# Causal attention with a convolved and a mixing feed-forward block: one-piece eviction of even heads, earlier inversion, held-back last products, one tap on ScalarE

## What is computed

```
cum    = cumsum(max(s, 0))
scores = q k^T / 8 + min(-(cum_i - cum_j), 0), causal mask, minus the row's maximum
x      = exp(scores) / (sum(exp(scores)) + 1e-9) @ v      heads side by side: 576 x 512
h      = relu(x @ w_in)                                    512 -> 1024
c      = conv_w[0]*h[t-1] + conv_w[1]*h[t] + conv_w[2]*h[t+1]
x1     = (h * sigmoid(c)) @ w_out                          1024 -> 512
u      = x1 + (U V)^T x1 over positions                    rank 32
out    = u + relu(u @ w_ch1) @ w_ch2                       512 -> 2048 -> 512
```

## Time and profile before

| | |
|---|---|
| median of 3 runs | 909.75 us (909.56 to 910.51) |
| profiled execution, its own time | 910.62 us |
| its span | 908.8 us |
| PE busy | 861.6 us, 95% |
| DVE, ACT, POOL busy | 468.5, 372.5, 50.6 us |
| granted clock of PE, mean | 0.992 |
| DMA | 150.36 MB, 165 GB/s |

### The profile page before, as it was taken

The page is one execution under the profiler, slowest core; times in us unless marked ns, Lnnn a source line. Parts: engine busy times, 40 slices in busy tenths (PEclk is TensorE's granted clock), DMA queues, the critical chain, the costliest instruction groups (busy, mean ns, idle before and its releaser), DMA issues.

```text
span 908.8 us, 15655 instructions
## 1 busy us (share of the span) xinstructions
PE 861.6 (95%) x6184; PEld 809.2 (89%) x6184; DVE 468.5 (52%) x984; ACT 372.5 (41%) x709; POOL 50.6 (6%) x105
## 2 busy tenths in 40 slices
PE   4888898989999999999999999999999999999998
PEld 3666888879998999889998999988999999999998
DVE  6788694464445934555344871455323761442222
ACT  2777675554425634544332653444221431221110
POOL 3021000000000000000000000000000000000000
PEclk9999998989999999999999999999999999999999
DMA  7686945636663557336545454435444444274441
GB/s 162 164 228 157 305 141 189 222 73 199 214 209 104 188 167 259 127 106 212 180 152 177 129 172 145 134 100 184 146 145 169 141 174 150 94 240 182 150 175 53
DMA packets 64396, 150.36 MB, mean 165 GB/s; under 512 B 30026, under 2 KB 44362, under 8 KB 51780
## 3 DMA queue, kind: packets, MB, share of 16 engines
q1 hardware_dynamic: 61252, 144.50, 49.4%
q0 software_dynamic: 3072, 4.87, 2.1%
HBM read 119.15 MB, written 30.11 MB: 164 GB/s over the span
## 4 chain that ended last, share of the span: by engine, by line
PE 66%; DVE 13%; issue 10%; ACT 5%; DMA 4%; POOL 1%; SPq 1%; DVEq 0%; ACTq 0%; POOLq 0%
PE psum L1190 18%; PE psum L1192 18%; PE psum L1191 17%; PE psum L1169 5%; DVE work L958 2%; DVE psum L899 2%; PE psum L1116 2%; DVE work L961 2%; DMA few_scratch<-few 2%; PE psum L1148 2%; PE psum L1146 2%; DMA spread_out<-few_scratch 2%; DVE work L956 1%; ACT work L746 1%; DVE ybuf L973 1%
## 5 line engine op out<-in xcount | busy, mean ns | idle before, releaser
L1190 PE MATMUL psum<-r_hl,ring 128*128 128x288 f32 x512 | 153.6, 300 | 3.2 <-DVE r_hl L1001 1.7
L1190 PE MATMUL psum<-uu_hl,ring 128*128 128x288 f32 x512 | 153.2, 299 | 1.5 <-DVE r_hl L1001 1.5
L1192 PE MATMUL psum<-r_hl,ring 128*128 128x288 f32 x512 | 151.2, 295 | 0.0
L1191 PE MATMUL psum<-r_hl,ring 128*128 128x288 f32 x512 | 151.1, 295 | 0.0
L1192 PE MATMUL psum<-uu_hl,ring 128*128 128x288 f32 x512 | 151.0, 295 | 0.0
L1191 PE MATMUL psum<-uu_hl,ring 128*128 128x288 f32 x512 | 150.9, 295 | 0.0
L783 ACT ACTIVATE r_hl<-psum 128x288 fp32r<-128x288 f32 x128 | 52.5, 411 | 188.1 <-PE psum L1192 188.0
L1001 DVE SCALAR_TENSOR_TENSOR r_hl<-psum,r_hl 128x288 fp32r<-128x288 f32 x128 | 58.5, 458 | 134.7 <-ACT r_hl L783 134.6
L1169 PE MATMUL psum<-probs,va 128*65 128x320 f32 (+4 forms) x448 | 109.6, 364 | 6.5 <-ACT probs L694 6.3
L899 DVE CUSTOM_DVE_ANT_0 psum<-psum,key_late 128x512 f32<-128x512 f32 (+4 forms) x160 | 84.9, 564 | 57.1 <-PE psum L1116 56.8
L1190 PEld LDWEIGHTS psum<-r_hl,ring 128*128 128x128 f32 x512 | 96.6, 189 | 5.5 <-DVE u_acc L1013 2.7
(11 more groups left out here) (101 smaller groups left out, 1626.6 us busy)
## 6 DMA issues: line engine op xcount, KB each, us to landing
ring<-w_scratch SPq DMA_DIRECT2D x74, 1024.0 KB, 4.9
w_scratch<-ring SPq DMA_DIRECT2D x24, 1024.0 KB, 6.1
kq_raw<-in_kq_t SPq DMA_DIRECT2D x64, 288.0 KB, 5.0
stage<-in_w_ch SPq DMA_DIRECT2D x16, 512.0 KB, 4.7
spread_out<-few_scratch POOLq DMA_DIRECT2D x32, 144.0 KB, 3.2
out_t<-u_acc SPq DMA_DIRECT2D x16, 288.0 KB, 3.7
va<-in_v SPq DMA_DIRECT2D x32, 128.0 KB, 2.8
stage<-in_w_out SPq DMA_DIRECT2D x4, 512.0 KB, 6.5
```

The lines of the kernel that those rows point to most:

```text
L1190: pe.matmul(o, hi, m_hi, start=start, stop=False)
L1191: pe.matmul(o, hi, m_lo, start=False, stop=False)
L1192: return pe.matmul(o, lo, m_hi, start=False, stop=stop)
```

## The change

Four parts.

1. **Eviction.** The even head's 65 rows are evicted in one instruction, with a bias column `eps_col` that holds 1e-9 in row 64 alone. Its sums then lie in row 64 of `x_raw`, which belongs to the odd head's half, and are gathered from there. So the odd head's ACT copy into `x_raw` now waits until the even head's gather has landed (`few_in`, 16 of 32). The odd head's gather waits for that too. At the steps of `EVICT_LATE` the eviction stands behind the group's feed-forward items.
2. **Inversion.** The last pair of batches 1 to 3 is inverted at the end of its own head 7, and for batches 1 and 2 normalised and split one step sooner. In batches 1 to 3 pair 1 is normalised at head 6, g = 1 instead of head 5, g = 3, and split at head 7 instead of head 6.
3. **Last products.** The first wi, wo and up of a batch do all tiles but the last for both halves, then the last tile of half 0, then (as the second item) that of half 1.
4. **Middle tap.** In batch 0 ACT makes the middle tap, right behind the second half of `hidden`; DVE makes the outer two.

```diff
-        X_SPLIT = [{(5, 0): 0, (7, 0): 1}, {(4, 0): 0, (6, 0): 1}]
-        X_SPLIT_LAST = [{}, {(0, 2): (NPAIR - 2,), (1, 0): (NPAIR - 1,)}, {(0, 0): (NPAIR - 2,), (0, 2): (NPAIR - 1,)}]
-        NORMALISE = [(4, 6), (3, 5, 7)]
-        INVERT_LAST = [(0, 1), (0, 0)]
-        NORMALISE_LAST = [(0, 4), (0, 1)]
+        EVICT_LATE = {(a, h) for a in PLAN for h in range(H - 1)
+                      if any(x[0] in ("turn", "rank", "mix") for x in PLAN[a][GROUPS * h + GROUPS - 1])}
+        X_SPLIT = [{(5, 0): 0, (7, 0): 1}, {(4, 0): 0, (7, 0): 1}]
+        X_SPLIT_LAST = [{}, {(0, 2): (NPAIR - 2,), (1, 0): (NPAIR - 1,)}, {(0, 0): (NPAIR - 2,), (0, 1): (NPAIR - 1,)}]
+        NORMALISE = [{(4, 2): 0, (6, 2): 1}, {(3, 3): 0, (6, 1): 1, (7, 3): 2}]
+        NORMALISE_LAST = [(0, 4), (0, 0)]
...
                 def gather_sums(a, h):
                     x = h % 2
-                    pool.wait_ge(evict.sem, evict.value(a * H + h, 1))
-                    row = sums[D * (1 - x):D * (1 - x) + 1, h // 2 % 2, :]
+                    n, m = a * H + h, a * NPAIR + h // 2
+                    if x:
+                        pool.wait_ge(few_in.sem, few_in.value(m, 16))
+                    pool.wait_ge(evict.sem, evict.value(n, 1) if x else evict.value(n))
+                    row = sums[0:1, h // 2 % 2, :] if x else x_raw[D:D + 1, h // 2, :]
...
                 def evict_head(a, h):
                     mm_pv.wait(act, n)
+                    if h % 2 == 0:
+                        xl_done.wait(act, m - NPAIR)
+                        act.activation(x_raw[0:D + 1, h // 2, :], psf[0:D + 1, O0:O0 + S], ACT.Identity, bias=eps_col[0:D + 1, :])\
+                           .then_inc(evict.sem, 2)
+                        return
                     if m >= 2:
                         few_in.wait(act, m - 2)
-                    act.activation(sums[sm:sm + 1, h // 2 % 2, :], psf[D:D + 1, O0:O0 + S], ACT.Identity, bias=EPS)\
+                    act.activation(sums[0:1, h // 2 % 2, :], psf[D:D + 1, O0:O0 + S], ACT.Identity, bias=EPS)\
                        .then_inc(evict.sem, 1)
-                    xl_done.wait(act, m - NPAIR)
-                    act.activation(x_raw[o:o + D, h // 2, :], psf[0:D, O0:O0 + S], ACT.Copy).then_inc(evict.sem, 1)
+                    few_in.wait(act, m, 16)
+                    act.activation(x_raw[D:2 * D, h // 2, :], psf[0:D, O0:O0 + S], ACT.Copy).then_inc(evict.sem, 1)
...
+                def middle_tap(b, f):
+                    m = b * FT + f
+                    relu.wait(act, b, 2 * f + 2)
+                    yl_done.wait(act, m - 2)
+                    act.activation(conv[f % 2], hid[:, f % 2, 1:S + 1], ACT.Copy, scale=cw[:, 1, f:f + 1]).then_inc(cv.sem, 1)
...
                     if kind == "wi":
                         hidden(b, i, half)
+                        if half and not b:
+                            middle_tap(b, i)
...
-                    dve.tensor_scalar(conv[i], hid[:, i, 1:S + 1], cw[:, 1, f:f + 1], None, ALU.mult).then_inc(cv.sem, 1)
+                    if b:
+                        dve.tensor_scalar(conv[i], hid[:, i, 1:S + 1], cw[:, 1, f:f + 1], None, ALU.mult).then_inc(cv.sem, 1)
...
-                    if a and (h, g) == INVERT_LAST[a > 1]:
-                        invert_few(a - 1, NPAIR - 1)
+                    if (a, h, g) == (1, 0, 1):
+                        invert_few(0, NPAIR - 1)
+                    if a and (h, g) == (H - 1, 4):
+                        invert_few(a, NPAIR - 1)
...
+                def first_products(item, tiles, m_hi, m_lo, ready):
+                    if item[-1] == 0:
+                        other = (*item[:-1], 1)
+                        products(item, tiles, m_hi, m_lo, ready, range(tiles - 1))
+                        if BEFORE[other]:
+                            evicted(BEFORE[other])
+                        products(other, tiles, m_hi, m_lo, None, range(tiles - 1))
+                    return products(item, tiles, m_hi, m_lo, ready, range(tiles - 1, tiles))
```

More of the change, by code:

```diff
@@ L131, in attention_and_ffn_program @@
         probs = sb("probs", [P, 2, BANK], F32)
+        eps_col = sb("eps_col", [P, 1], F32)
         row_max = sb("row_max", [P, 8], F32R)
@@ L170, in attention_and_ffn_program @@
         w_stored = [Count(sem(f"w_stored{i}"), 16) for i in range(RING)]
-        s_ident, s_mask, s_zero, s_rows, s_rows1, s_hid, s_va = (sem(n) for n in ("s_ident", "s_mask", "s_zero", "s_rows", "s_rows1", "s_hid", "s_va"))
+        s_ident, s_mask, s_zero, s_rows, s_rows1, s_hid, s_va, s_eps = (sem(n) for n in ("s_ident", "s_mask", "s_zero", "s_rows", "s_rows1", "s_hid", "s_va", "s_eps"))
         s_relu, s_scan, s_cumh, s_cuml, s_uvh, s_uvl = (sem(n) for n in ("s_relu", "s_scan", "s_cumh", "s_cuml", "s_uvh", "s_uvl"))
@@ L628, in _ @@
                 pool.memset(uv_stage[:, :, :], 0.0).then_inc(s_zero, 1)
+                pool.wait_ge(s_zero, 1)
+                pool.memset(eps_col[:, :], 0.0).then_inc(s_eps, 1)
+                pool.wait_ge(s_eps, 1)
+                pool.memset(eps_col[D:D + 1, :], EPS).then_inc(s_eps, 1)
                 def gather_sums(a, h):
                     x = h % 2
-                    pool.wait_ge(evict.sem, evict.value(a * H + h, 1))
-                    row = sums[D * (1 - x):D * (1 - x) + 1, h // 2 % 2, :]
+                    n, m = a * H + h, a * NPAIR + h // 2
[3 more added lines that the diff above has]
+                    row = sums[0:1, h // 2 % 2, :] if x else x_raw[D:D + 1, h // 2, :]
                     pool.dma_start(few[0][x * D:(x + 1) * D, :], row).then_inc(few_in.sem, 16)
@@ L718, in attention_step @@
                         prepare_queries(a, h + 2)
-                    if g == 4:
+                    if g == 4 and (a, h) not in EVICT_LATE:
                         evict_head(a, h)
@@ L732, in then @@
                         prepare_queries(a, h + 2)
+                    if g == 4 and (a, h) in EVICT_LATE:
+                        evict_head(a, h)
                 def hidden(b, f, half):
@@ L833, in _ @@
                 max_to_row(0, 0)
+                act.wait_ge(s_eps, 2)
                 for h, g in ATT_STEPS:
@@ L838, in _ @@
                 act.wait_ge(s_hid, 1)
+                act.wait_ge(cw_in, 48)
                 bodies(body_step, ffn_step, then)
@@ L936, in then @@
                         invert_few(a, h // 2 - 1)
-                    if g == 2 + (a > 0) and h in NORMALISE[a > 0]:
-                        normalise_few(a, NORMALISE[a > 0].index(h))
+                    if (h, g) in NORMALISE[a > 0]:
+                        normalise_few(a, NORMALISE[a > 0][h, g])
                     if g == 2 and a:
@@ L1215, in evicted, with products @@
                         acc.wait(pe, b, NTH[item] + 1)
-                def products(item, tiles, m_hi, m_lo, ready=None):
+                def products(item, tiles, m_hi, m_lo, ready=None, ks=None):
                     half = item[-1]
                     hi, lo = weights(item)
-                    for k in range(tiles):
+                    for k in ks or range(tiles):
                         if ready:
@@ L1230, in wi @@
                     x_ready = lambda k: xl_done.wait(pe, b * NPAIR + k)
-                    products(item, KT, *x_hl, x_ready if f == 0 and half == 0 else None).then_inc(mm_wi.sem, 1)
+                    (products(item, KT, *x_hl) if f else first_products(item, KT, *x_hl, x_ready)).then_inc(mm_wi.sem, 1)
                 def wo(item):
@@ L1235, in wo @@
                     y_ready = lambda k: yl_done.wait(pe, b * FT + k)
-                    products(item, FT, *y_hl, y_ready if d == 0 and half == 0 else None).then_inc(mm_wo.sem, 1)
+                    (products(item, FT, *y_hl) if d else first_products(item, FT, *y_hl, y_ready)).then_inc(mm_wo.sem, 1)
                 def turn(b, t, half):
@@ L1266, in up @@
                     u_ready = lambda k: ul.wait(pe, b, k + 1)
-                    products(item, KT, *uu_hl, u_ready if unit == 0 and f == 0 and half == 0 else None).then_inc(mm_up.sem, 1)
+                    (products(item, KT, *uu_hl) if unit or f else first_products(item, KT, *uu_hl, u_ready)).then_inc(mm_up.sem, 1)
                 def down(item):
```

5 lines of the change are left out of this document (1 added, 4 removed).

## The result

The changed kernel takes 930.06 us (median of 6 runs, 928.3 to 932.62) against 909.65 us (6 runs of the kernel before on the same chip): ratio 1.0227, 95% interval 1.0207 to 1.0248. It is slower, as forecast, but by 20.4 us instead of 6; the forecast of 915.7 and its range up to 921 are missed. The profiled execution took 932.62 us, its span 930.8.

A forecast was written before the change was run, and what follows sets the result against it. PE, busy 95%, was taken as the bound. Profiled 910.62 us + 13.9 (waits and clock) - 7.9 (gains) = 916.6, or 915.7 at the runs' median; own range 911 to 919, with rivals 905 to 921.

The forecast's parts named there:

- the first wait: Batch 0: odd heads' ACT copies wait for the even head's gather; head 3 6.1 us, head 5 1.7, head 7 2.8.
- The clock: PE's clock falls behind the batch 0 stalls: 2.2 us lost for head 3, 1.1 for head 7, nothing for head 5.
- rival C: Clock costs more: all three stalls drop it at 2.7 us each, or it stays low a whole head; 920.5 us, chance 0.11.
- Batch 1's wi: Earlier inversion removes the 1.18 us wait at 281.27; the shorter even-head eviction at 289.5 helps too: 2.0 us gained.
- Batch 2's wi: First wi of batch 2, 1.67 us idle and 1.84 late: 1.8 us gained.
- Middle taps: Batch 0's wi: eight taps leave DVE for ACT; net 0.6 us gained, between -1.0 and 3.6.
- Late eviction: In the turns, a turned tile's copies go before sums and x_raw; PE's 1.50 us wait at 182.56 shrinks by 0.9.
- Reordered products: Last tile held back: batch 0's first wi loses its 0.80 us wait, 1.3 us gained in all there; reordered wo 0.
- Even evictions: Batch 0: three times 0.66 us leave ACT, but DVE paces each head: 0 gained; if not, 1.
- A: Gathers land quickly, head 2's after 1.7 us: added waits 3.2 us in all, kernel faster at 905 us; chance 0.15.
- B: The odd heads' waits for the gather are covered and only the gains stay: 902 us; chance 0.07.
- D: ACT becomes the chain in batch 0's wi, half of eight taps on the path, 2.7 us more: 919 us; chance 0.07.

The follow-up runs named there:

- experiments 1, 3, 4: Changed kernel, last normalise one step later: 916.1 us; with old eviction too: 904.14. Kernel before with new inversion/normalise/split timetable alone: 919.89; with early inversion alone: 904.54.
- both_back_tap_on_vector: `both_back` with batch 0's middle tap again on VectorE: 903.57 us, ratio 0.9941 to the kernel before.
- both_back: Changed kernel with the old eviction and gather, and the last pair's normalise of batches 1 and 2 one step later: 904.14 us, ratio 0.9947 to the kernel before.

## Why the prediction missed

*Direction and the first wait: right.* The wait was found by the forecast's own reading: head 3 6.35 us (6.1 forecast), head 5 2.33 (1.7), head 7 3.48 (2.8), the first exponentials of head 4 at 57.08 ("near 57"). The clock fell behind all three stalls, not two, so rival C's mechanism held. Batch 0's one-piece eviction as a whole cost 15 to 16 us (916.1 against 901.2 and 900.18), where 13.9 were forecast. In the trace the first exponentials fall back by 6.3 us over head 3's wait (6.1 forecast), by 3.2 more up to head 6 (3.9: 2.2 of clock and head 5's 1.7), by 4.7 up to head 0 of batch 1 (2.8: head 7's wait, no clock), and by 2.6 up to its head 2 (1.1 of clock). So the clock was priced too high at head 3, from two intervals of the first head in which the clock column itself said 1.00, and too low at the other two; that the sum came within 1 to 2 us is in part luck. Its 10 matmuls "in 2 us" at the low level were in fact 10 in 1.71 us, PE's busy time in that window; the factor of 10/18 holds all the same, by the up products' 0.24 us against 0.13.

*Where it failed: the terms "Batch 1's wi" (2.0) and "Batch 2's wi" (1.8).* The forecast said that "the inversion stands four r_hl and a group of maxima sooner, so that the normalised pair is there before the wi". It asked what a sooner normalised pair would give, and not when the normalise could run. The timetable moved the inversion by one step and the normalise with it, and the forecast held nothing against the time of the two DMAs between them: 8.5 us from inversion to normalise in the kernel before. It also took no account of the place where the inversion now falls, right behind a ring block and two kq_raw loads, nor of r_hl, queued behind the normalise on both engines. In place of a gain of 3.8 the runs show a cost of 13 to 15 us for these two lines (experiments 1, 3, 4): 10.3 us of idle PE, and its slow clock behind. The changed kernel without the two lines takes 916.1 us, and the forecast was 915.7: they are all but about 1 us of the error of 14.4. The trace agrees within 1.6: the exponentials fall back by 4.4 and 4.6 us there, where the forecast had them catch up 2.0 and 1.8, 12.8 in all. Without the lines the terms come out nearly as forecast: those of the three batches were 5.1, of which 0.8 was for the even head's eviction at 289.5, and the early inversion alone gives 3.6 to 3.8 of the other 4.3.

*The small terms.* Middle taps 0.6 gained: nothing in the run times, and about 1 us of new idle time in the trace, at the lower bound that the forecast had given (-1.0). It had seen one delayed exponential, near 111, and priced it at 0.6; there are two, of 1.2 and 0.8. Late eviction 0.9: the wait meant fell by 0.8, but the one-piece eviction alone takes nearly as much from it. Reordered products: 0.85 gained at batch 0's first wi, 0.60 lost at the first up, a place that the forecast left out. Even evictions 0 in batch 0: agreed, 901.2 us with them there and 900.18 without, so no gain. In batches 1 to 3 they are worth about 3 us; the forecast had two of the three waits behind them, at 92.38 (inside its 1.3 for the first wi of batch 0) and at 292.74 (the 0.8 above), and not the one near 130.

*The rivals.* A's short landing was not it: 6.6 us at head 2. B was refuted by the stalls. D came in small: two exponentials were held by taps on ACT, and PE lost 1.1 us net, not 2.7. No rival had the normalise as a wait, though the diff shows its line; this was the one that would have reached 930.

## What to carry to other kernels

When an operation that needs a DMA's result moves in an in-order queue, write down three times: when the DMA can start, how long it takes behind the transfers issued just before it, and what is queued behind the operation that will wait. Moving the producer and the consumer by the same step gains nothing for the consumer. And before a wait for a small DMA is called the DMA's, look at its issuing queue: here 7.7 of the 14 us between eviction and landing were GpSimd's order, mended by issuing the gather one place sooner and the memset one pair later.

## What the runs showed of the hardware

A store of 4.5 KB landed after 1.8 us with the loads held back, after 4.1 with a block of 1 MB issued 1.3 us before it by another engine, and after 6.9 with 1.6 MB issued around it; the spread of 2 x 144 KB landed after 2.8 us with the loads held back and after 5.3 behind a block of 1 MB. A column operand on ScalarE costs a little. These two groups of the changed kernel are the gate's tanh, whose scale is a constant, and the column-scaled tap, of the same shape; the plain copies of that shape take 670 to 685 ns.

```profile
L772 ACT ACTIVATE work<-work 128x576 f32<-128x576 f32 x32 | 21.9, 684 | 22.3 <-DVE work L994 22.1
...
L765 ACT ACTIVATE work<-hid,cw 128x576 f32<-128x576 f32 x8 | 6.2, 778 | 0.3
```

94 ns more, where the Trainium skill (ScalarE: Activation LUTs, What ACT_TABLE_LOAD costs) has about 93.

PE's clock does not answer the same stall in the same way each time. Behind the wait for row maxima at the end of batch 0's wi, 2.88 us in the kernel before and 2.87 in `both_back_tap_on_vector`, it fell in the one profiled execution and held in the other (first row before, second row that kernel):

```profile
140.00:144.00 4.00, 3.71 (x18) 0.50 0.33 133
```
```profile
138.00:142.00 4.00, 3.43 (x29) 1.00 0.25 98
```

The wait of 2.27 us at the same place was followed by 0.59 in the changed kernel (156 to 160) and by 1.00 in `both_back` (142 to 146). So a term for the clock behind a stall of 2 to 3 us is a chance, not a price.
